# A fused attention and two-layer kernel: its first block of tokens reordered, eight more weight splits on GpSimd

## The reference

```python
def _attn_ref(q, k, v):                       # q, k, v: (8, 8, 576, 64)
    k_p = k.reshape(B, H, Sp, pool, D).mean(axis=3)      # pool = 8, Sp = 72
    v_p = v.reshape(B, H, Sp, pool, D).mean(axis=3)
    scores = scale * np.matmul(q, k_p.transpose(0, 1, 3, 2))
    scores = scores - np.max(scores, axis=-1, keepdims=True)
    attn = np.exp(scores)
    attn = attn / (np.sum(attn, axis=-1, keepdims=True) + 1e-09)
    return np.matmul(attn, v_p).astype(np.float32)

def _moe_ref(x, w_in, w_out):                 # w_in 512x2048, w_out 2048x512
    h = x @ w_in
    g = np.where(pos, h, np.where(neg, 0.0, (h + beta) ** 2 / (4.0 * beta)))   # beta = 1
    return (g @ w_out).astype(np.float32)

def _moe2_ref(x, w_in, w_out):
    h = x @ w_in
    g = h * (1.0 / (1.0 + np.exp(-h)))
    return (g @ w_out).astype(np.float32)
```

## Time and profile before

| | us |
|---|---|
| median of 3 runs | 1725.03 |
| profiled execution, whole | 1725.77 |
| its span, first to last instruction | 1724.0 |
| TensorE busy | 1681.4 (98% of the span) |
| VectorE, ScalarE, GpSimd busy | 692.6, 509.1, 535.8 |
| mean granted TensorE clock | 0.993 of full speed |

### The profile page before, as it was taken

The page is one execution under the profiler, slowest core; times in us unless marked ns, Lnnn a source line. Parts: engine busy times, 40 slices in busy tenths (PEclk is TensorE's granted clock), DMA queues, the critical chain, the costliest instruction groups (busy, mean ns, idle before and its releaser), DMA issues.

```text
span 1724.0 us, 20982 instructions
## 1 busy us (share of the span) xinstructions
PE 1681.4 (98%) x7568; PEld 1358.6 (79%) x7568; DVE 692.6 (40%) x919; ACT 509.1 (30%) x856; POOL 535.8 (31%) x407
## 2 busy tenths in 40 slices
PE   6699999999999999999999999999999999999998
PEld 4567777787777778778887888888888888888887
DVE  5585747567464756642355321212121212121211
ACT  4333233232322323232344332322232223222221
POOL 5443433434253443522222222222222222222221
PEclk9899999999999999999999999999999999999999
DMA  7364443425243443420123110101010101000000
GB/s 181 89 170 122 99 108 96 118 76 114 88 112 102 96 118 76 126 63 27 43 86 116 49 50 0 49 0 49 0 49 0 48 0 42 7 34 15 24 0 24
DMA packets 139797, 114.96 MB, mean 67 GB/s; under 512 B 86676, under 2 KB 95892, under 8 KB 139764
## 3 DMA queue, kind: packets, MB, share of 16 engines
q1 hardware_dynamic: 136884, 109.28, 23.4%
q10 hardware_dynamic: 2880, 5.24, 1.0%
HBM read 74.65 MB, written 39.85 MB: 66 GB/s over the span
## 4 chain that ended last, share of the span: by engine, by line
PE 47%; issue 33%; POOL 13%; DVE 4%; ACT 2%; DMA 0%; POOLq 0%; SPq 0%; ACTq 0%; DVEq 0%
PE ps_y L588 8%; PE ps_y L589 8%; PE ps_y L590 8%; PE ps_h L588 8%; PE ps_h L590 8%; PE ps_h L589 8%; POOL g_lo L1070 6%; POOL kv_raw L277 5%; DVE g_tmp L993 1%; DVE wout_lo L904 1%; POOL v_sum L277 1%; DVE g_tmp L986 1%; DVE prob L932 0%; ACT g_tmp L794 0%; DVE row_den L927 0%
## 5 line engine op out<-in xcount | busy, mean ns | idle before, releaser
L1070 POOL TENSOR_TENSOR g_lo<-g_tmp,g_hi 128x512 fp32r<-128x512 f32 x288 | 373.6, 1297 | 1135.7 <-ACT g_hi L801 1135.7
L588 PE MATMUL ps_h<-x_hi,win_hi 128*128 128x512 f32 x1144 | 451.5, 395 | 1.9 <-DVE win_lo L904 1.8
L590 PE MATMUL ps_h<-x_hi,win_lo 128*128 128x512 f32 x1144 | 446.0, 390 | 0.0
L589 PE MATMUL ps_h<-x_lo,win_hi 128*128 128x512 f32 x1144 | 445.9, 390 | 0.0
L997 DVE TENSOR_TENSOR g_tmp<-g_tmp,ps_h 128x512 f32<-128x512 f32 x144 | 99.1, 688 | 579.5 <-ACT g_tmp L791 579.5
L588 PEld LDWEIGHTS ps_h<-x_hi,win_hi 128*128 128x128 f32 x1144 | 214.8, 188 | 60.6 <-issue 13.8
L801 ACT ACTIVATE g_hi<-g_tmp 128x512 fp32r<-128x512 f32 x288 | 182.4, 633 | 231.5 <-DVE g_tmp L993 125.8
L590 PEld LDWEIGHTS ps_h<-x_hi,win_lo 128*128 128x128 f32 x1144 | 215.0, 188 | 45.2
L589 PEld LDWEIGHTS ps_h<-x_lo,win_hi 128*128 128x128 f32 x1144 | 215.2, 188 | 43.2
L588 PE MATMUL ps_y<-g_hi,wout_hi 128*128 128x512 f32 x576 | 230.0, 399 | 13.4 <-DVE g_tmp L993 11.6
L589 PE MATMUL ps_y<-g_lo,wout_hi 128*128 128x512 f32 x576 | 226.3, 393 | 0.0
(11 more groups left out here) (105 smaller groups left out, 1238.3 us busy)
## 6 DMA issues: line engine op xcount, KB each, us to landing
p_dram<-x_raw SPq DMA_DIRECT2D x28, 384.0 KB, 2.3
kv_raw<-in_k_dram SPq DMA_DIRECT2D x16, 576.0 KB
y_dram<-y_sb SPq DMA_DIRECT2D x36, 256.0 KB, 2.1
x_raw<-y_dram SPq DMA_DIRECT2D x18, 512.0 KB, 4.4
out_dram<-y_sb SPq DMA_DIRECT2D x36, 256.0 KB, 2.1
kv_raw<-in_v_dram SPq DMA_DIRECT2D x15, 576.0 KB
x_raw<-x_dram SPq DMA_DIRECT2D x16, 512.0 KB, 4.2
q_pair<-in_q_dram SPq DMA_DIRECT2D x120, 64.0 KB, 5.0
```

The lines of the kernel that those rows point to most:

```text
L588: mm(dst, w_h, a_h, start=first, stop=False)
L589: mm(dst, w_h, a_l, start=False, stop=False)
L590: return mm(dst, w_l, a_h, start=False, stop=last)
L1070: nc.gpsimd.tensor_tensor(g_lo[:, s % G_BUFS, :], g_tmp[:, s % T_BUFS, :], g_hi[:, s % G_BUFS, :].bitcast(F32), ALU.subtract).then_inc(g_l ...
```

## The change

It touches the first block of layer 1 most, and one table entry for all blocks.

- The first batch: VectorE pools the keys of pairs 0 and 1 only, GpSimd those of pair 2 first of all its work. `first_scores(3)` moves ahead of `first_values(1)`, and `first_hidden` is cut into halves that stand on both sides of `first_probs` of pairs 2 and 3. On ScalarE two exponentials, and on VectorE the transpose of the tail queries and `split_low(8)`, change places with their neighbours.
- The gates of steps 0 to 3 are begun one behind the other, with no attention slot between them, and TensorE does hidden(4) and hidden(5) ahead of the tail's scores and output(0). Slot 0 (tail scores) is now in step 4, slots 1 to 5 in step 5, slots 6 to 10 in step 6; from step 7 on the slots stand where they stood. The tail's values (slot 7) move behind hidden(6).
- GpSimd makes the low parts of pieces 16 to 19 and 24 to 27 as well, behind `gate_low` and the attention slots of their step. Pieces 9 to 15 keep VectorE, in other steps; pieces from 16 on are split in step 6 and later, two per step (16 and 17 in step 6, 18 and 19 in step 7, 26 and 27 in step 11). Before, 18 and 19 were split in step 6, and 26 and 27 in step 10.
- In all blocks Q stands at slot 5u + 2 and no longer at 5u + 3.

```diff
-PIECES = {2: [("K", 0)], 3: [("Q", 0)]}
+PIECES = {2: [("K", 0), ("Q", 0)]}
...
-        PIECES.setdefault(5 * _u + 3, []).append(("Q", _u))
+        PIECES.setdefault(5 * _u + 2, []).append(("Q", _u))
...
-FIRST_SLOTS = [[], [0], [1], [2], [3, 4], [5, 6, 7, 8]]
+FIRST_SLOTS = [[], [], [], [], [0], [1, 2, 3, 4, 5]]
...
+        if s == AHEAD + 2:
+            return [6, 7, 8, 9], [10]
         return [2 * s - 3], [2 * s - 2]
...
-        POOL_PIECES = 8
+        POOL_LOADS = list(range(8)) + list(range(16, 20)) + list(range(24, 28))
...
+        REST_LOADS = [[], [], [9], [10], [11, 12], [13, 14, 15]]
         def rest_loads(s):
-            if s < 3:
-                return [FIRST_LOADS + s]
-            at = FIRST_LOADS + 3 + 2 * (s - 3)
-            return range(at, min(at + 2, W_PIECES))
+            at = 16 + 2 * (s - AHEAD - 2)
+            return REST_LOADS[s] if s < AHEAD + 2 else range(at, min(at + 2, W_PIECES))
...
             def first_block():
+                hidden(0, AHEAD, 0)
+                hidden(0, AHEAD + 1, 0)
                 attention_slot(0, 0, UNITS)
-                hidden(0, AHEAD, 0)
                 output(0, 0, 0, 0)
                 output(0, 1, 0, 0)
-                hidden(0, AHEAD + 1, 0)
                 attention_slot(0, 2, UNITS)
                 output(0, 2, 0, 0)
                 attention_slot(0, 5, UNITS)
                 output(0, 3, 0, 0)
-                attention_slot(0, 7, UNITS)
...
-            for c in range(PAIRS):
+            for c in range(2):
                 first_probs(c)
-                if c + 2 < PAIRS:
-                    first_keys(c + 2)
-                    first_queries(c + 2)
+                first_keys(c + 2)
+                first_queries(c + 2)
+                if c == 0:
+                    first_values(c)
+                first_scores(c + 2)
+                if c == 1:
+                    first_values(c)
+            for c in range(2, PAIRS):
+                first_hidden(c - 2, 0, 2)
+                first_probs(c)
+                first_hidden(c - 2, 2, AHEAD)
                 first_values(c)
...
             first_exp(0)
-            first_queries(1)
+            first_exp(1)
             first_probs(0)
-            first_exp(1)
...
             dve.wait_ge(w_lo_pool, 7)
-            split_low(8)
-            one_block(0, 0, UNITS, loads=rest_loads)
+            gate_begin(0, 0)
+            gate_begin(0, 1)
+            gate_end(0, 0, 0)
+            gate_end(0, 1, 0)
+            one_block(0, 0, UNITS, loads=rest_loads, first=True)
...
                     gate_low(B, s)
                     for slot in behind if pooling else ():
                         attention_slot(B, slot)
+                    for n in rest_loads(s) if isinstance(B, int) and B == 0 else ():
+                        if n in POOL_LOADS:
+                            split_low(n)
```

More of the change, by code:

```diff
@@ L235, in wait_split @@
         def wait_split(eng, n):
-            if n < POOL_PIECES:
-                eng.wait_ge(w_lo_pool, n + 1)
+            of_pool = sum(m <= n for m in POOL_LOADS)
+            if n in POOL_LOADS:
+                eng.wait_ge(w_lo_pool, of_pool)
             else:
-                eng.wait_ge(w_lo_done, n - POOL_PIECES + 1)
+                eng.wait_ge(w_lo_done, n + 1 - of_pool)
         def load_weight(eng, n):
@@ L693, in first_values, with first_hidden @@
                 pair_values(early_o[c], c, pT_early)
-            def first_hidden(c):
-                wait_split(pe, c)
-                pe.wait_ge(x_lo_done, c + 1)
-                for s in range(AHEAD):
+            def first_hidden(c, low, high):
+                if low == 0:
+                    wait_split(pe, c)
+                    pe.wait_ge(x_lo_done, c + 1)
+                for s in range(low, high):
                     last = hidden_chunk(first_bank[s], s, c)
@@ L813, in one_block @@
             def one_block(B, layer, units=0, loads=lambda s: (), more=True, first=False):
-                for s in range(FC):
+                for s in range(2 if first else 0, FC):
                     before, behind = slots_of(B, s)
@@ L871, in _ @@
             first_queries(3)
+            first_probs(1)
+            first_exp(3)
             first_input(1)
@@ L1009, in copy_y, with one_block @@
                                           ).then_inc(y_copied_dve, 1)
-            def one_block(B, layer, units=0, loads=lambda s: (), more=True):
-                for s in range(FC):
+            def one_block(B, layer, units=0, loads=lambda s: (), more=True, first=False):
+                for s in range(2 if first else 0, FC):
                     before, behind = slots_of(B, s)
@@ L1021, in one_block @@
                     for n in loads(s):
-                        split_low(n)
+                        if n not in POOL_LOADS:
+                            split_low(n)
                 if more:
@@ L1029, in _ @@
             dve.wait_ge(pad_zero, 1)
-            for c in range(3):
+            for c in range(2):
                 pool_early(dve, c, 0)
@@ L1096, in _ @@
             split_low(1)
+            split_low(2)
             pool_early(pool, 3, 1)
-            split_low(2)
-            split_low(3)
-            for n in range(4, POOL_PIECES):
+            for n in range(3, 8):
                 split_low(n)
```

39 lines of the change are left out of this document (23 added, 16 removed).

## The result

The changed kernel takes 1729.48 us (median of 7, 1726.27 to 1731.41), the kernel before on the same chip 1724.03 (median of 7, 1723.35 to 1725.66). The ratio is 1.0026 with a 95% interval of 1.0016 to 1.0036: slower, by more than noise; whether by more than the 0.2% at which the prediction draws its line, the interval leaves just open. Forecast were 1727.3 us, within 1719.0 to 1732.0. The median lies 1 us above 1728.5, where the prediction's own "slower" (0.36) begins, and not within the 0.2% that it gave the largest chance (0.42).

A forecast was written before the change was run, and what follows sets the result against it. TensorE was taken as busy nearly throughout except in the first 86 us; its lead ran 6.4, 0.65, -0.95, -4.55, -2.25, so 1725.77 became 1728.1, less 0.74 for the median: 1727.3 us, range 1719.0 to 1732.0.

The forecast's parts named there:

- Part 1: First block up to the first pair's scores: they start at 71.6 instead of 78.02, 6.4 us sooner.
- S1: The first pair's scores on TensorE in the first block; forecast to start at 71.6, between 69.0 and 74.5.
- lead: How many us earlier the new kernel reaches a point of TensorE's order; forecast 6.4 at the first pair's scores, -2.25 at the end.
- Part 2: From S1 to hidden(8): 28.35 us instead of 22.6, waiting for GpSimd's splits of pieces 18 and 19; 1.6 more for clock.
- S4: The fourth pair's scores, which TensorE makes last before hidden(12); taken at 1.25 us.
- Part 3: At hidden(12): pieces 26 and 27 are split behind the fourth pair's exponential; 6.7 us from S4 instead of 3.07, loss 3.6.
- Part 4: Blocks 1 to 7: queries transposed a slot sooner, so six waits for them go, a gain of 2.3 us.
- The sum: Whole kernel: about 2.3 us slower, 1725.77 to 1728.1 for the profiled execution; median 0.74 lower, 1727.3.
- The rule weighed: GpSimd's eight added splits block the SBUF port twice as long as on VectorE; without the rule, 2.9 us lower, near 1724.5.
- (a): Rival at hidden(8): GpSimd has pieces 18 and 19 split by the end of the first pair's values; 1720.6 us, chance 0.22.
- (b): Rival near 50 us: piece 9's split meets the second key half's landing, gate 4 near 60; 1730.2 us, chance 0.26.
- (c): Rival in the later blocks: turning queries sooner does nothing, the six waits stay; 1729.6 us, chance 0.10.

The follow-up runs named there:

- e4: Changed kernel with VectorE's low part of piece 8 moved behind the last tile's input: 1730.93 us, ratio 1.0032 to the kernel before.
- e2: Changed kernel with the queries turned at slot 5u+3 again: 1733.97 us, ratio 1.0047 to the kernel before.
- e10: Changed kernel with the splits of steps 8 to 11 moved up, 26 and 27 in step 10: 1725.30 us, ratio 0.9995 to the kernel before.
- e12: Changed kernel with batch 1's second key half pooled a step later and piece 8 split last on VectorE: 1729.62 us, ratio 1.0018.
- e5: Changed kernel with the splits ahead of the attention slots on ScalarE and GpSimd from step 6 on: 1727.16 us, ratio 1.0010.
- e1: Kernel before with only the queries turned at slot 5u+2 instead of 5u+3, in all blocks: 1722.03 us, ratio 0.9981.
- e6: Changed kernel with the low parts of pieces 16 to 19 and 24 to 27 back on VectorE, in the same steps: 1728.72 us, ratio 1.0020.

## Why the prediction was right, and where

**Part 1, S1.** Forecast 71.6, measured 72.38, and the lead of 6.4 was 5.6. The chain was the right one (issue at 47.86 for 46.2, second half worked from 53.30 for 50.4), but two of its terms failed, by 3.7 and 2.9 us, and cancelled by luck. Gate 4 began at 60.81, not 57.1: 1.7 us for the later issue, 1.2 for the landing, and 1.1 for the split of piece 10, which took 2.42 beside the two `g_lo`, less 0.3 for shorter pooling. It fell there because ScalarE's copy of the piece stands behind `gate_high(3)`, which waited for output(0) until 57.29. And the tail's division, for which I had taken 4.9 with a double collision, met nobody and took 2.0. That TensorE's being sooner in the first batch decides nothing is shown by e4. Two waits stand nowhere in the prediction: 1.63 us at hidden(3), behind a split that took VectorE 4.11 us, and 4.56 us at 64.46, where K waits for the take. Both lie ahead of S1 in TensorE's order, which is why they cost nothing further; still, "a wait that stands nowhere above" was one of the prediction's own signs of being wrong.

**Part 2, hidden(8).** Forecast 28.35 us from S1 and a wait of about 5, then 1.6 us of clock. In the profiled execution: 27.47, a wait of 5.38, and from hidden(8) to S4 1.6 us lost. Here the mechanism was right in each piece. The size was right for only one of two ways through steps 5 to 7. In the four other profiled executions that have the changed kernel's splits in steps 5 to 7, behind the slots (e2, e4, e10, e12), it took 30.97, 30.99, 30.93 and 28.16: three of five above my upper bound of 30.0. Two terms were too small there. "From the begin of gate 7 to `gate_low` 5.9" measured 5.6 us in the changed kernel and in e12, but 7.9 to 8.2 in e2, e4 and e10: from `row_den` to the end of the product it is 1.9 one way and 4.2 to 4.5 the other. And "S1 and output(3), 5.65" measured 5.5 in the first two and 6.6 in the other three, where TensorE's clock stayed at the 1.2 GHz level longer behind S1 (0.57 in e10's slice from 76 to 78, 0.99 in the changed kernel's). So of the 3.5 us between the changed kernel and e10, 1.1 arise ahead of step 7. The spread of the changed kernel's own times (three at 1726.3 to 1728.1, four at 1729.5 to 1731.4) fits two ways some 3 us apart, but only one of those executions has a trace, and before spreads by as much (1722.62 to 1727.92 in 27), so this is argued, not shown.

**Part 3, hidden(12).** Forecast a wait of 5.4 and a loss of 3.6; measured 5.44 and 3.5. e10 takes it away and gains 5 us. The sum of hand-overs named the exponential as the one to wait for; e5 adds that GpSimd's queue would have made it 4.5 without it. What the part missed is 0.8 us behind it: "the clock falls at this place in both", but it is low for 5.3 us, where it was for 3.3, and block 1's tail scores are 5.2 behind, not 4.55.

**Part 4, Q.** Forecast 2.3 us; from block 1's tail scores to the end the lead rises by 3.8. e1 and e2 give 3.2 and 3.6 for the whole kernel, but 1.4 of e1's gain lies in the first block. The waits for queries behind the first block sum to 2.2 us in the kernel before and in e2, and are gone in e1 and in the changed kernel, as forecast. The step priced a wait by its idle time alone. Five of the six are short, like this one; before, and then now:

```profile
372.13 1.24 PE L529 MATMUL ps_a<-kT,qT 128*128 128x144 f32 x8 [0.24 <-DVE qT L949]
```

```profile
375.74 1.14 PE L532 MATMUL ps_a<-kT,qT 128*128 128x144 f32 x8
```

From the tail's scores of this block to those of the next it was 99.07 us (361.97 to 461.04), and now it is 98.53 (365.99 to 464.52): 0.5 us for a wait of 0.24. The scores behind the wait are 0.1 slower; the rest shows in no wait of TensorE and stays open. And 0.5 of the 3.8 us come behind block 7, in layer 2, where no queries are turned.

**The sum.** Forecast 2.3 us slower for the profiled execution, measured 1.7; but 5.5 by the medians. The step that failed is the last: "The median of the runs is 0.74 lower than that execution", carried over to a kernel whose own profiled execution is 2.0 below its median. That the profiled executions agree with the forecast within 1 us is luck in part: counted in lead, part 1 came out 0.8 us worse than forecast, part 2 0.9 better, part 3 0.7 worse and part 4 1.5 better.

**The rule weighed.** That VectorE's two-input instructions and GpSimd's exclude each other was borne out several times (2.42 us at 58.47, where 0.69 is usual); `row_den`, which has one input, was held up as well (1.30 for 0.17). The conclusion drawn from it was too coarse. Where the collisions fall decides, and that the eight splits moved to GpSimd is not what made the change slow: with them back on VectorE (e6) it is as slow within about 1 us.

**Rivals.** (a), that GpSimd keeps up, is out by the wait of 5.38. (b), one collision near 50 us, came in part: gate 4 at 60.81 is its "near 60", by a later landing and a collision at 58.5 instead, and S1 was saved by the missing one in step 5. (c) is out by e1.
